# Interleaving the state transposes with the state's part of y, and a unit's first products between up and down

## The reference

```
for t in range(S):
    y[:, :, t] = einsum('bhd,bhde->bhe', rt, state)
    Sa = einsum('bhde,bhe->bhd', state, at)
    state = state * wt[:, :, None, :] - einsum('bhd,bhe->bhde', Sa, bt) + einsum('bhd,bhe->bhde', vt, kt)
x = y as (3072 tokens, 320)
x = leaky_relu(x @ w_in) @ w_out                    # 320 -> 2048 -> 320
x = sigmoid(x @ w_gate) * (x @ w_val) @ w_out2      # 320 -> 1536 -> 320
```

## Time and profile before

| | |
|---|---|
| time of the kernel, 3 runs | 1124.49, 1126.1, 1138.29 us |
| profiled execution: span from first to last instruction (no other time of it is listed) | 1129.2 us |
| TensorE busy | 1072.3 us, 95% |
| VectorE busy | 595.8 us, 53% |
| ScalarE busy | 397.3 us, 35% |
| GpSimd busy | 146.4 us, 13% |
| mean granted TensorE clock | 0.973 of full |

### The profile page before, as it was taken

The page is one execution under the profiler, slowest core; times in us unless marked ns, Lnnn a source line. Parts: engine busy times, 40 slices in busy tenths (PEclk is TensorE's granted clock), DMA queues, the critical chain, the costliest instruction groups (busy, mean ns, idle before and its releaser), DMA issues.

```text
span 1129.2 us, 36605 instructions
## 1 busy us (share of the span) xinstructions
PE 1072.3 (95%) x16106; PEld 917.0 (81%) x16106; DVE 595.8 (53%) x1306; ACT 397.3 (35%) x782; POOL 146.4 (13%) x179
## 2 busy tenths in 40 slices
PE   2888979999999999999999999999999999999998
PEld 2777868888888887788788788888888888888887
DVE  7797786767676776667574224443223232323222
ACT  2142243344444443533343335542222222222222
POOL 6313030403122121303010000000000000000000
PEclk9977679999999999999999999999999999999999
DMA  5836363344335342434333024220201002020000
GB/s 176 252 103 151 68 129 80 82 110 123 85 75 134 89 108 62 125 90 100 64 110 79 9 91 145 80 89 1 61 1 57 5 1 61 1 61 1 24 1 23
DMA packets 133856, 87.62 MB, mean 78 GB/s; under 512 B 98274, under 2 KB 113634, under 8 KB 133700
## 3 DMA queue, kind: packets, MB, share of 16 engines
q1 hardware_dynamic: 126740, 62.85, 22.8%
q0 software_dynamic: 6960, 22.45, 6.6%
HBM read 66.39 MB, written 18.87 MB: 76 GB/s over the span
## 4 chain that ended last, share of the span: by engine, by line
PE 89%; issue 4%; DVE 3%; ACT 1%; POOL 1%; DMA 0%; SPq 0%; ACTq 0%; POOLq 0%; DVEq 0%
PE bank L808 16%; PE bank L858 12%; PE pair L858 12%; PE bank L823 4%; PE bank L878 4%; PE bank L876 4%; PE bank L877 4%; PE bank L824 4%; PE bank L825 4%; PE bank L894 3%; PE bank L783 2%; PE bank L760 2%; PE bank L774 2%; PE bank L630 2%; PE bank L828 2%
## 5 line engine op out<-in xcount | busy, mean ns | idle before, releaser
L1301 DVE TENSOR_TENSOR g_lo<-g_full,g_hi 128x512 fp32r<-128x512 f32 x168 | 125.3, 746 | 229.8 <-ACT g_hi L1064 229.6
L1064 ACT CAST g_hi<-g_full 128x512 fp32r<-128x512 f32 x168 | 104.3, 621 | 134.7 <-DVE g_full L1354 131.6
L808 PE MATMUL bank<-x_hi,w_up 128*128 128x512 f32 x480 | 134.7, 410 | 3.6 <-issue 3.6
L1057 ACT ACTIVATE g_full<-bank 128x512 f32<-128x512 f32 x96 | 57.5, 599 | 210.0 <-PE bank L808 204.7
L1256 DVE TENSOR_TENSOR t_unit<-t_unit,prod 128x126 f32<-128x126 f32 (+22 forms) x372 | 106.5, 286 | 12.8
L1252 DVE TENSOR_TENSOR prod<-t_unit,p_unit 128x126 f32<-128x126 f32 (+22 forms) x372 | 102.1, 275 | 20.1 <-DMA p_unit<-p_dram 7.0
L808 PEld LDWEIGHTS bank<-x_hi,w_up 128*128 128x128 f32 x480 | 85.4, 189 | 23.0 <-issue 4.5
L1354 DVE TENSOR_TENSOR g_full<-pair,h_sb 128x512 f32<-128x512 f32 x36 | 24.9, 692 | 112.7 <-PE pair L858 112.0
L808 PE MATMUL bank<-x_lo,w_up 128*128 128x512 f32 x288 | 82.1, 393 | 0.0
L823 PE MATMUL bank<-g_hi,w_dn 128*128 128x512 f32 x192 | 76.4, 398 | 0.4 <-DVE g_lo L1301 0.2
L824 PE MATMUL bank<-g_hi,w_dn 128*128 128x512 f32 x192 | 75.0, 391 | 0.0
(11 more groups left out here) (146 smaller groups left out, 2401.0 us busy)
## 6 DMA issues: line engine op xcount, KB each, us to landing
p_unit<-p_dram SPq DMA_DIRECT2D x48, 128.0 KB, 2.9
stage<-in_w_out POOLq DMA_DIRECT2D x7, 640.0 KB, 5.8
v_tok<-in_vT SPq DMA_DIRECT2D x12, 320.0 KB, 3.1
v_nu<-in_vN SPq DMA_DIRECT2D x24, 160.0 KB, 5.9
x<-y_sb SPq DMA_DIRECT2D x48, 80.0 KB
k_sb<-in_kF POOLq DMA_DIRECT2D x22, 160.0 KB, 3.4
v_sb<-in_vF SPq DMA_DIRECT2D x22, 160.0 KB
r_sb<-in_rF SPq DMA_DIRECT2D x22, 160.0 KB
```

The lines of the kernel that those rows point to most:

```text
L808: last = nc.tensor.matmul(up_bank(m)[:], lhs, rhs, start=(e == 0), stop=(e == len(products) - 1))
L1064: nc.scalar.copy(g_hi[:, m % 2], g_full[:]).then_inc(g_hi_ready, 1)
L1301: nc.vector.tensor_tensor(g_lo[:, m % 2], g_full[:], g_hi[:, m % 2].bitcast(F32), ALU.subtract).then_inc(g_lo_ready, 1)
```

## The change

`pe_sn` and `pe_y_begin` become one function, `pe_y_begin_sn`: for each q it issues two products of y for chunk n and two transposes of the state for chunk n+1. For that, y's products write the other half of the partitions (input rows of half i, output in half 1-i), `pe_y_end` likewise, and `dve_y` copies each half by itself with the halves exchanged. The transposes' bank is now 4 for the first chunk of a unit and 7 for the second; `act_sn` follows in step 3 ahead of `act_rhs`, and in step 6. The transposes are gone from steps 0 and 4. `first` of chunk n = 2 g moves from the end of step 0 to step 1, between `up` and `down`, and its copy `act_first` to step 1, behind `act_g` (and behind `act_x` where there is one).

```diff
-        BANKS = dict(rhs=((4, 5), (4, 5)), sn=((6,), (6,)), first=((7,), (7,)), a=((6,), (6,)), ka=((7,), (7,)),
+        BANKS = dict(rhs=((4, 5), (4, 5)), sn=((4,), (7,)), first=((7,), (7,)), a=((6,), (6,)), ka=((7,), (7,)),
...
-        TENSOR_ORDER = [("rhs", 0, 0), ("sn", 0, 0), ("first", 0, 0),
...
+        TENSOR_ORDER = [("rhs", 0, 0),
+                        ("first", 0, 0), ("a", 2, 0), ("ka", 1, 0), ("ut", 0, 0), ("u", 0, 0),
...
-        def pe_sn(pe, n):
+        def pe_y_begin_sn(pe, n):
+
             u, c = divmod(n, 2)
-            claim(pe, "sn", n)
-            wait(pe, state_ready, n if c else n - 2)
-            o = bank[bank_of("sn", n)]
+            nxt = n + 1
+            if unit_in(u) and n >= 0:
+                claim(pe, "y", n)
+                emptied(pe, "sn", n)
+            if unit_in(nxt // 2):
+                claim(pe, "sn", nxt)
+                wait(pe, state_ready, nxt if nxt % 2 else nxt - 2)
+                o_sn = bank[bank_of("sn", nxt)]
+            o_y = bank[bank_of("y", n)]
             for q in range(TQ):
-                for i in range(2):
-                    last = nc.tensor.matmul(o[half(i, D), q * D:(q + 1) * D], st_sb[half(i, D), u % 2, q],
-                                            ident[half(i, D), half(i, D)], start=True, stop=True)
-            last.then_inc(bank_filled[bank_of("sn", n)], 1)
+                if unit_in(u) and n >= 0:
+                    for i in range(2):
+                        nc.tensor.matmul(o_y[half(1 - i, D), q * L:(q + 1) * L], sn_sb[half(i, D), q],
+                                         r_sb[half(i, D), c, q], start=(q == 0), stop=False, skip_group_check=True)
+                if unit_in(nxt // 2):
+                    for i in range(2):
+                        last = nc.tensor.matmul(o_sn[half(i, D), q * D:(q + 1) * D], st_sb[half(i, D), nxt // 2 % 2, q],
+                                                ident[half(i, D), half(i, D)], start=True, stop=True)
+            if unit_in(nxt // 2):
+                last.then_inc(bank_filled[bank_of("sn", nxt)], 1)
...
-                    if s == 6 and now:
-                        pe_y_begin(pe, n + 1)
-                        pe_y_end(pe, n + 1)
+                    if s == 1 and now:
+                        pe_first(pe, n)
+                        fill(pe, "first", n)
+                    elif s == 6 and (now or soon):
+                        pe_y_begin_sn(pe, n + 1)
+                        if now:
+                            pe_y_end(pe, n + 1)
...
                         pe_rhs_end(pe, n)
-                        pe_sn(pe, n)
                         fill(pe, "sn", n)
-                        pe_first(pe, n)
-                        fill(pe, "first", n)
...
-                        pe_y_begin(pe, n)
+                        pe_y_begin_sn(pe, n)
...
                             pe_ut_u(pe, n + 1)
-                            pe_sn(pe, n + 1)
...
         def act_sn(act, n):
             filled(act, "sn", n)
-            multiplied(act, "y", n - 1)
...
                         act_rhs(act, n)
-                        act_sn(act, n)
-                        act_first(act, n)
...
                         if now:
+                            act_first(act, n)
                             act_cross(act, n)
...
+                        act_sn(act, n + 1)
                         act_rhs(act, n + 1)
...
-            nc.vector.tensor_tensor(y_sb[:], bank[bk][:].rearrange("p (q t) -> p q t", t=L), decay[:, n % 6, :, 0:L],
-                                    ALU.mult).then_inc(bank_emptied[bk], 1)
+            for i in range(2):
+                last = nc.vector.tensor_tensor(y_sb[half(i)], bank[bk][half(1 - i)].rearrange("p (q t) -> p q t", t=L),
+                                               decay[half(i), n % 6, :, 0:L], ALU.mult)
+            last.then_inc(bank_emptied[bk], 1)
```

More of the change, by code:

```diff
@@ L214, in unit_in @@
             return 0 <= u < NU
-        BANKS = dict(rhs=((4, 5), (4, 5)), sn=((6,), (6,)), first=((7,), (7,)), a=((6,), (6,)), ka=((7,), (7,)),
+        BANKS = dict(rhs=((4, 5), (4, 5)), sn=((4,), (7,)), first=((7,), (7,)), a=((6,), (6,)), ka=((7,), (7,)),
                      ut=((4,), (4,)), u=((5,), (5,)), st=((5,), (5,)), vrur=((6, 7), (6, 7)), y=((6,), (6,)),
                      kb=((4, 7), (5, 6)))
-        TENSOR_ORDER = [("rhs", 0, 0), ("sn", 0, 0), ("first", 0, 0),
-                        ("a", 2, 0), ("ka", 1, 0), ("ut", 0, 0), ("u", 0, 0),
+        TENSOR_ORDER = [("rhs", 0, 0),
+                        ("first", 0, 0), ("a", 2, 0), ("ka", 1, 0), ("ut", 0, 0), ("u", 0, 0),
                         ("st", 0, 0), ("vrur", 0, 0),
-                        ("rhs", 0, 1), ("y", 0, 0), ("first", 0, 1),
-                        ("a", 2, 1), ("ka", 1, 1), ("ut", 0, 1), ("u", 0, 1), ("sn", 0, 1),
+                        ("rhs", 0, 1), ("y", 0, 0), ("sn", 0, 1), ("first", 0, 1),
+                        ("a", 2, 1), ("ka", 1, 1), ("ut", 0, 1), ("u", 0, 1),
                         ("st", 0, 1), ("vrur", 0, 1),
-                        ("y", 0, 1),
+                        ("y", 0, 1), ("sn", 1, 0),
                         ("kb", 1, 0), ("kb", 1, 1)]
@@ L765, in pe_vrur @@
                         last.then_inc(bank_filled[6 + i], 1)
[L767 to L775, removed]
         def pe_y_end(pe, n):
@@ L782, in pe_y_end @@
                 for i in range(2):
-                    last = nc.tensor.matmul(o[half(i, D), q * L:(q + 1) * L], kb_tok[:, c, i, q],
+                    last = nc.tensor.matmul(o[half(1 - i, D), q * L:(q + 1) * L], kb_tok[:, c, i, q],
                                             vrur(i)[:, q], start=False, stop=(q == TQ - 1), skip_group_check=True)
@@ L1167, in scalar_program @@
                             act_ut(act, n + 1)
-                            act_sn(act, n + 1)
-                    elif s == 6 and later and g >= 2:
-                        act_t_unit(act, g + 2)
+                    elif s == 6 and soon:
+                        act_sn(act, n + 2)
+                        if later and g >= 2:
+                            act_t_unit(act, g + 2)
                     elif s == 7:
```

## The result

| | median | runs | ratio to before, 95% interval |
|---|---|---|---|
| before | 1129.37 us | 20 | |
| changed | 1123.12 us | 20 | 0.9943 [0.9925, 0.9961] |

The change makes the kernel faster by 0.57%, 6.4 us (4.4 to 8.5). The forecast was 11.7 us less.

A forecast was written before the change was run, and what follows sets the result against it. TensorE's stream was taken to bound the kernel. Terms 4.0 + 7.2 + 4.2 - 2.2 - 0.8 - 0.7 = 11.7 us of gain, from the three-run median 1126.1, gave 1114.4 us, range 1103 to 1126.

The forecast's parts named there:

- What bounds the kernel: From about 165 us on, TensorE has hardly a hole; time saved there comes off the end unless another engine delays it.
- Step 4, 1.20 a unit: `ut`/`u` to next `up` falls from 2.24 to 1.04 without transposes and their wait: 1.20 in six units, 7.2 in all.
- The new block at 0.99: Interleaved y and transposes in steps 3 and 6 take 0.99, like `a` with `ka`; costs 2.2 and 0.8 us.
- The rule of 60 cycles a matmul: Counter-argument: 25 ns a record would make the new block 1.6 us and the sum some 14 us worse; not followed.
- The copy of y: On VectorE, 24 copies become 48 of 0.69, 16.6 us more; only one, ahead of unit 2, costs the path 0.7.
- Steps 0 and 1, 4.0 of gain: Without waits 9.42 becomes 8.84; gains 2.8 in units 4, 6, 8 and 1.2 in 9 and 11, together 4.0 us.
- Units 0 to 2, nothing: Steps 0 and 1 there gain nothing: the first solve or GpSimd's chain sets the pace, TensorE's saving becomes idle time.
- The one that other queues take the gain of steps 0 and 1: `cross` waits in odd units too, or y copies push `g_lo`: 4.0 lost, 1118.4, or 1122 with more; chance 0.17.
- The no-overlap rival: New block's parts don't overlap: steps 3 and 6 cost 17.0 in place of 3.0, time 1128.4; chance 0.08.
- Slower, by the clock: More idle TensorE in units 0 to 2 adds half-clock stretches, about 7 us lost each; chance 0.09.

The follow-up runs named there:

- e6_split_copy: The kernel before with only y's copy on VectorE split into two halves of 64 partitions; ratio to before 0.9994.
- e3_interleave_only: The changed kernel with `first` and its copy back in step 0, directly behind `rhs`; ratio to before 0.9947.
- e2_first_only: The kernel before with only the move of `first` and its copy to step 1, transposes and y as before; ratio to before 1.0076.
- e4_same_half: The changed kernel with y's products and copy in their old half, sharing the transposes' quarters of the array; ratio to before 1.0060.
- e5_glo_early: The changed kernel with `act_first` between `act_g` and `act_x`, and three of six inverse columns moved behind `g_lo`; ratio to before 0.9871.

## Why the prediction was half right

1. **What bounds the kernel**: right. Behind unit 2 the end moved with TensorE's stream, and the tail from unit 11's `rhs` stayed at 502 us in every kernel.
2. **Step 4, 1.20 a unit**: right, from 2.24 to 1.04 in units 3 to 6, within 0.03 in all but one place. From `ut` to `up`, 10.6 us were won over nine units, 9.3 forecast. Some of the surplus is pauses that have moved on to another place of the stream: in units 7 to 9 before had 2.7 there and the changed kernel has 0.9 to 1.5, but it has pauses in `ut` of units 7 and 8 in step 1, and in `first` of units 3, 4 and 11 in step 3.
3. **The new block at 0.99**: its size was off, to my disadvantage. It takes what y took alone, 0.81 and 1.02; 3.0 us of cost in the sum were not there. The row taken for it, `a` with `ka`, was no bound. The rule of 60 cycles a matmul (the Trainium skill, "TensorEngine Tiling (Array Packing)", Performance Considerations) does not hold as a price for each record here: 32 records of y alone take the 25 ns each that I had estimated from it, but 64 in four quarters, in the same 0.81, 13 ns each.
4. **The copy of y**: right in kind (48 of 688 ns), nearly nothing on the path, shown by e6_split_copy.
5. **Steps 0 and 1, 4.0 of gain: this step failed.** The nine units took 1.4 more than before, not 4.0 less. The block lengths held (8.86 to 8.96 in units without waits, 8.84 forecast), as did the 0.57 of `cross` in unit 4. Without waits the nine units would take 79.6 (8.86 eight times, 8.69 for unit 11), 5.1 less than before's 84.7 (9.43 eight times and 9.25). But the waits and pauses grew from 3.9 (88.6 - 84.7) to 10.4 (90.0 - 79.6). The table below splits them up. The waits for other engines, 5.2 together, came to what I had priced, 5.5, though in other units: `g_lo` held up units 3, 5 and 9 in the first profile, unit 9 in the second and none in the third, where units 3, 5 and 7 had been priced. What failed is that I put everything else at nothing. TensorE's own stream was to run without a pause, since it had done so in these steps before; the runs show 2.4 to 4.1 us of pauses inside `ut` of units 7, 8 and 9, and `a` and `ut`, or an `up`, at half clock. Outside these steps the same two made step 2 longer by 1.0, and pauses in `first` of step 3 made the +2.4 of their row. The pauses come with the move of `first`: all ten profiles with it have more of them than any of the four without, e3_interleave_only among these, and the experiments agree. The move alone made the kernel 0.76% slower, and without it the interleaving was as fast as the whole change.
6. **Units 0 to 2, nothing.** The timed executions speak against it: by the mean clock, up to 4.6 us of the gain were lost to more time at half clock. e2_first_only, e3_interleave_only and e4_same_half have 0.975 to 0.976 against 0.980 of the kernel before on the same chip, and e6_split_copy, which leaves TensorE's order alone, is not below it (0.980, before 0.977 on its chip). So it seems to come with a new order on TensorE. Against that, e5_glo_early (five executions) has 0.978 and before 0.977 on its chip. Which wait is behind it no run tests.
7. **The rivals.** The one that other queues take the gain of steps 0 and 1 gave nearly the time, with 7.7 us of gain left by its sum and 6.4 measured, but that is luck. `cross` did not wait in odd units and y's copies did not push `g_lo` (e6_split_copy), which were its two reasons. The no-overlap rival is refuted by the block. "Slower, by the clock" came true in part, as in 6, on top of a smaller gain. The profiled executions would have said the opposite (34, 48 and 41 us at half clock up to unit 2, before's 58 and 55); the many timed ones make that look like chance.

The waits and pauses in steps 0 and 1 of point 5, in the mean of the profiles:

| wait or pause, units 3 to 11, us | before | changed | priced in the forecast |
|---|---|---|---|
| `cross` for `u_first` | 0 | 2.6 | 2.2 (0.55 in four units) |
| `down` for `g_lo` | 0.3 | 1.3 | 3.3 (1.09 in three units) |
| `up` for `x_lo` | 2.1 | 0.6 | 0 |
| `a` for GpSimd | 0 | 0.7 | 0 |
| pauses inside `ut` | 0 | 3.0 | 0 |
| the rest: short gaps, half-clock stretches | 1.5 | 2.2 | 0 |

What stays open is what the pauses inside blocks wait for; the instruction transfers are the one partner that the profiles offer. They often come at the same places of TensorE's stream (inside `up` of unit 6, inside `ut` of unit 8) and last 0.3 to 3.2 us.

## What to carry to other kernels

Before a block is taken out of a stream, look at what it covered: the 0.91 of transposes in step 0 hid a copy and was worth nothing, the 0.74 in step 4 hid nothing and, with its own wait, was worth 1.20. When TensorE is made to arrive earlier at a point where several engines' chains meet, count its gain only down to the next of these chains, and put a small consumer's copy ahead of bulk copies in the same queue. Here two groups of small products merged for nothing when they used different quarters of the array, and for nearly their full price (0.62 of 0.74) when they did not. Compare the clock over all timed executions, not only in the profiled one: here the profiled ones had it the wrong way round.

## What the runs showed that I had not expected

- 32 transposes of 40x40 issued between 32 records of y, in the other two quarters of the array, added 0.00 to 0.01 us to y's 0.81; in the same quarters they added 0.62.
- An order on GpSimd that starts one scaling earlier cost 10 to 11 parts in a thousand, twice, though the wait it was made for disappeared. TensorE waited 6.1 and 6.7 us for another load in unit 1, and its mean clock fell from 0.975 and 0.978 to 0.968 and 0.969.
- Half-clock stretches of 3.4 us, once 6.8, in the middle of dense work (unit 6, 8 or 9), right behind idle times of 0.9 to 3.2 us of TensorE; one makes an `up` or the products of `a` and `ut` take nearly twice their time.
- 80 pauses of TensorE inside blocks, each ending 2.1 to 3.1 us after the start of an instruction transfer on DMA queue 8.
